# Splits moved on GpSimd and ScalarE, one load moved ahead, and the new part's weights in four groups of 32 columns from round 7 on

## The reference, cut to what matters

```
for t in range(768):                      # attention with a decaying state, B=2, H=8, D=48
    y[t]  = r[t] @ (state + (u*k[t]) v[t]^T)
    state = w[t][:,None]*state + k[t] v[t]^T
h = gelu(x @ w_in); u, v = halves of h    # stage 2, x is y as [2, 768, 384]
x1 = x + (u * (w_sg @ norm(v)*g_ln + b_sg)) @ w_out
x2 = x1 + (relu(x1^T @ tok1) @ tok2)^T    # stage 3
out = x2 + relu(x2 @ ch1) @ ch2
```

## Time and profile before

| what | us |
|---|---|
| time, median of 3 runs | 368.2 (368.17 to 368.8) |
| the profiled execution's own time | 369.53 |
| its span, first to last instruction | 368.0 |
| PE busy in the span | 359.9 |
| POOL busy | 188.6 |
| DVE busy | 163.0 |
| ACT busy | 106.6 |
| the six `xT` jobs that begin TAIL start at | 86.47 |

### The profile page before, as it was taken

One profiled execution on the slowest core, in us unless ns is written; L12 is line 12 of the kernel. 1 busy time (PEld: TensorE's weight loads), 2 busy tenths in 40 slices (PEclk: granted clock), 3 DMA queues, 4 the chain that ended last, 5 costly groups with the idle time before them and its releaser, 6 DMA issues.

```text
span 368.0 us, 6598 instructions
## 1 busy us (share of the span) xinstructions
PE 359.9 (98%) x2620; PEld 322.8 (88%) x2620; DVE 163.0 (44%) x272; ACT 106.6 (29%) x205; POOL 188.6 (51%) x191
## 2 busy tenths in 40 slices
PE   8999898999999999999999999999999999999996
PEld 8788787998999999999999998888888888888885
DVE  7989886656203323583469443340033300233100
ACT  3876267546450044310121312330022200132000
POOL 5997999999684465779999940037000000000000
PEclk9999999999999999999999999999999999999999
DMA  7985993311122000021223400000000000000011
GB/s 239 412 289 183 369 381 114 109 45 45 43 90 83 3 1 0 2 86 45 86 87 128 128 2 0 2 2 28 30 28 0 2 28 28 30 0 0 2 47 38
DMA packets 12463, 29.78 MB, mean 81 GB/s; under 512 B 1680, under 2 KB 5904, under 8 KB 12432
## 3 DMA queue, kind: packets, MB, share of 16 engines
q1 hardware_dynamic: 12432, 29.35, 22.8%
HBM read 26.99 MB, written 2.36 MB: 80 GB/s over the span
## 4 chain that ended last, share of the span: by engine, by line
PE 84%; POOL 8%; issue 3%; DVE 3%; ACT 1%; DVEq 0%; POOLq 0%
PE bank L1269 25%; PE bank L1268 25%; PE bank L1270 25%; PE bank L1291 2%; PE bank L1355 2%; PE bank L1454 2%; POOL sg_lo L621 1%; PE bank L1400 1%; POOL rp L677 1%; POOL rku L640 1%; POOL yt L693 1%; POOL rku L632 1%; POOL rstd L703 1%; PE bank L1301 1%; PE bank L1333 1%
## 5 line engine op out<-in xcount | busy, mean ns | idle before, releaser
L902 ACT ACTIVATE ha_hi<-bank 128x512 fp32r<-128x512 f32 x36 | 21.6, 601 | 106.6 <-PE bank L1270 106.6
L1176 DVE SCALAR_TENSOR_TENSOR ha_lo<-bank,ha_hi 128x512 fp32r<-128x512 f32 x36 | 24.9, 692 | 50.6 <-ACT ha_hi L902 50.6
L1268 PE MATMUL bank<-ha_hi,c_lo 128*128 128x512 f32 x108 | 42.1, 390 | 0.0
L1270 PE MATMUL bank<-u2T_hi,c_hi 128*128 128x512 f32 x108 | 42.0, 389 | 0.0
L1269 PE MATMUL bank<-u2T_lo,c_hi 128*128 128x512 f32 x108 | 42.0, 389 | 0.0
L1270 PE MATMUL bank<-ha_hi,c_hi 128*128 128x512 f32 x108 | 42.0, 389 | 0.0
L1269 PE MATMUL bank<-ha_lo,c_hi 128*128 128x512 f32 x108 | 42.0, 389 | 0.0
L1268 PE MATMUL bank<-u2T_hi,c_lo 128*128 128x512 f32 x108 | 42.0, 389 | 0.0
L1268 PE MATMUL bank<-sg_hi,z_lo 128*128 128x384 f32 x96 | 32.1, 334 | 0.0
L1269 PE MATMUL bank<-sg_lo,z_hi 128*128 128x384 f32 x96 | 32.1, 334 | 0.0
L1270 PE MATMUL bank<-sg_hi,z_hi 128*128 128x384 f32 x96 | 32.1, 334 | 0.0
(11 more groups left out here) (144 smaller groups left out, 833.6 us busy)
## 6 DMA issues: line engine op xcount, KB each, us to landing
turned<-in_turned_all SPq DMA_DIRECT2D x9, 772.0 KB, 7.7
raw<-in_moe_w_ch SPq DMA_DIRECT2D x12, 384.0 KB, 3.1
rows<-in_rows_all SPq DMA_DIRECT2D x6, 576.0 KB, 7.0
raw<-in_moe_w_sg SPq DMA_DIRECT2D x6, 384.0 KB, 3.0
out<-x2T SPq DMA_DIRECT2D x8, 256.0 KB, 2.0
raw<-in_moe_w_in SPq DMA_DIRECT2D x4, 384.0 KB, 5.0
raw<-in_moe_w_tok SPq DMA_DIRECT2D x4, 384.0 KB, 3.2
rows<-in_rows_all SPq DMA_DIRECT2D x6, 192.0 KB, 5.5
```

The source lines that it names most:

```text
L902: sc.activation(ha[0][:, i, :], bank[:, :], ACT.Relu).then_inc(act_out, 1)
L1176: ve.scalar_tensor_tensor(ha[1][:, i, :], bank[:, :], 0.0, ha[0][:, i, :].bitcast(F32), ALU.max, ALU.subtract).then_inc(dve_out, 1)
L1268: te.matmul(dst, left[1], right[0], start=first, stop=False)
L1270: return te.matmul(dst, left[0], right[0], start=False, stop=last)
```

## The change

Six edits:

- SP: the load `rows` of chunk 6 goes out ahead of the raw load of piece 2 (w_in 0), no longer behind it.
- The scaled r of round 0: POOL makes pair 0 only and DVE pairs 1 to 3 (before two and two). The scores of round 0 go through the pairs in the order 1, 2, 3, 0.
- POOL's low parts: w_in 1 moves from chunk 7 to 8, w_sg 0 from 8 to 9, w_sg 1 from 9 to 10, w_sg 2 from 10 to the work after the rounds.
- In chunk 11 POOL's `rstd_tile` comes behind `diagonal_v`, and ACT's `normal` for the same tile moves from round 11 to behind the last `xT` of TAIL.
- ACT's high part of w_in 0 moves from the end of round 5 into round 6, behind its `xT` job.
- PE: from round 7 on the new part takes the masked scores in four groups of 32 columns, so a round has 64 instructions at this line.

```diff
             load_raw(1)
+            load_rows(6)
             load_raw(2)
-            load_rows(6)
...
-            low = {6: [("w_in", 0)], 7: [("w_in", 1)], 8: [("w_sg", 0)], 9: [("w_sg", 1)], 10: [("w_sg", 2)]}
+            low = {6: [("w_in", 0)], 8: [("w_in", 1)], 9: [("w_sg", 0)], 10: [("w_sg", 1)]}
...
-                if len(last) == 1:
+                early = len(last) == 1 and n < NCH - 1
+                if early:
                     rstd_tile(*last[0])
...
                 diagonal_v(n)
-                if len(last) > 1:
+                if not early:
                     for b, i in last:
                         rstd_tile(b, i)
...
-                for i in range(3, NC):
+                for i in range(2, NC):
                     split_low("w_sg", i)
...
+                if n == YR + 1:
+                    split_high("w_in", 0)
                 if n % NC < NC - 1:
                     take_state(n)
...
-                if len(last) == 1:
+                if len(last) == 1 and n < NCH - 1:
                     normal(*last[0])
...
+                if (kind, b, i) == ("xT", 1, NC - 1):
+                    normal(*v_jobs(NCH - 2)[0])
...
-                ve.tensor_tensor(rp[0:QP, 0, 2:NP, :], kr_tile(0, 1)[:, 2:NP, :], pre_tile()[:, 2:NP, :], ALU.mult
+                ve.tensor_tensor(rp[0:QP, 0, 1:NP, :], kr_tile(0, 1)[:, 1:NP, :], pre_tile()[:, 1:NP, :], ALU.mult
...
+            quarters = [tile(i, HP // 2) for i in range(4)]
...
-                    for q in halves:
+                    for q in quarters if n > YR + 1 else halves:
                         ins = te.matmul(y_bank(n)[q, tile(h, D)], am[:, h, q], v_row(n)[:, tile(h, D)],
```

More of the change, by code:

```diff
@@ L667, in scale_first_r @@
                 pool.wait_ge(pre0_half, 1)
-                gp.tensor_tensor(rp[0:QP, 0, 0:2, :], kr_tile(0, 1)[:, 0:2, :], pre_tile()[:, 0:2, :], ALU.mult
+                gp.tensor_tensor(rp[0:QP, 0, 0:1, :], kr_tile(0, 1)[:, 0:1, :], pre_tile()[:, 0:1, :], ALU.mult
                                  ).then_inc(rp0_half, 1)
@@ L936, in split_high @@
                 sc.copy(hi, raw_view(piece, hi)).then_inc(w_hi_act, 1)
-            high = {5: [("w_in", 0)], 6: [("w_in", 1)], 7: [("w_sg", 0)], 8: [("w_sg", 1)],
+            high = {7: [("w_sg", 0)], 8: [("w_sg", 1)],
                     9: [("w_sg", 2)]}
@@ L986, in _ @@
                     take_job(*job)
-                for piece in high[n]:
-                    split_high(*piece)
+            split_high("w_in", 1)
             for n in range(YR + 2, NCH):
@@ L1077, in scale_first_r @@
                 wait_r(dve, 0)
+                dve.wait_ge(pre0_half, 1)
                 dve.wait_ge(pre_done, 1)
-                ve.tensor_tensor(rp[0:QP, 0, 2:NP, :], kr_tile(0, 1)[:, 2:NP, :], pre_tile()[:, 2:NP, :], ALU.mult
+                ve.tensor_tensor(rp[0:QP, 0, 1:NP, :], kr_tile(0, 1)[:, 1:NP, :], pre_tile()[:, 1:NP, :], ALU.mult
                                  ).then_inc(rp_done, 1)
@@ L1285, in scores @@
                     pe.wait_ge(masked, 2 * n)
-                for p in (range(NP) if n else (2, 3, 0, 1)):
+                for p in (range(NP) if n else (1, 2, 3, 0)):
                     if n == 0 and p == 0:
```

## The result

The changed kernel takes 366.79 us (median of 5 runs, 366.53 to 366.94), the kernel before 368.8 beside it (5 runs, 368.17 to 369.44). The ratio is 0.9948, 95% interval 0.9935 to 0.9961: 1.9 us faster by the ratio, 2.0 between the medians. Forecast was 365.8, with a range of 364.4 to 368.6. The profiled execution took 366.67 us, its span is 365.1.

A forecast was written before the change was run, and what follows sets the result against it. PE was taken as the bound, by how early it reaches TAIL. Terms -0.95, -1.15, -0.41, 0 and 0 made -2.5 us, the new part -1.0 + 1.1: -2.4, from 368.2 to 365.8 us; range 364.4 to 368.6.

The forecast's parts named there:

- the splits: POOL's low parts one chunk later: the stop ahead of round 9's scores goes, gain 1.15 us.
- the load of rows 6: Issued ahead of raw piece 2, it shortens PE's stop in round 6; gain 0.95 us, between 0.5 and 1.2.
- What bounds it: PE holds 84% of the chain of waits; the question is how early it reaches TAIL; three stops total 2.78 us.
- The lower bound of 1.3 us: Least gain in the landing of rows 6: one long raw-load issue of 1.70 us against 0.37, about 1.3 us.
- rival D: Stops come back elsewhere: rows 6 gains too little or rows 10 comes late; half of 2.5 left, 367.0 us; chance 0.13.
- rstd and normal: Moved out of round 11: PE's wait ahead of TAIL's first v job goes, gain 0.41 us.
- Round 0 and ACT's split: DVE's larger product in round 0 and ACT's later split of w_in 0: taken as 0, round 0 within -0.2 and +0.2.
- The new part: Four groups side by side in rounds 7 to 11: -1.0 us; nine changes of tile shape at 0.12: +1.1 us.
- A: New part's four groups run only two by two: +2.6 us, 368.3 us in all; chance 0.17.
- B: Each new-part instruction still costs 28.8 ns: +4.6 us, 370.3 us, up to 371.4; chance 0.13.
- C: New part's four groups run side by side, with no price for the change of shape: 364.7 us; chance 0.20.

The follow-up runs named there:

- the second look: The kernel before, run and profiled again with no edit: 368.45 us, span 366.9; the new part of round 6 starts at 38.56.

## Why the prediction was right, and where not

The measured time lies in the range. What was gained came by the splits and the lead that they give POOL; the second largest term, the load of rows 6, had next to nothing behind it.

- *What bounds it.* Right: the time went by how early PE reached TAIL, and from there on both kernels run alike.
- *The load of rows 6, -0.95.* Wrong. "The load `rows` of chunk 6" was late in the execution profiled, not in the kernel: the second look, the edit undone (367.02) and the changed kernel all start the new part of round 6 at 38.6. Its worth by the undone edit is 0 to 0.2 us. The lower bound of 1.3 us failed too: the long second issue went over to the load of rows, which ended 0.2 us sooner. One execution of 369.53 us, 1.3 above its median, was the sign, and I used it only to shift the sum. That is the first condition of rival D (the load gains too little), and by the absolute time D's 367.0 is nearer to 366.79 than the forecast's 365.8. By the gain it is not: 2.0 us measured, 2.4 forecast, 1.25 in D.
- *The splits, -1.15.* Right: 1.1 by undoing it, and 62.93 - 61.79 = 1.14 in the start of round 9's scores. POOL's `rp` ended at 61.08, 0.7 ahead of them, 1.0 said.
- *rstd and normal, -0.41.* Right that the edit removes the stop, since it does so with the splits back in their old chunks. But the splits alone remove it too, by POOL's lead of 2 to 3 us, which the same text had worked out; so the edit adds nothing to them (366.73 with it undone). The size was 0.66 by the distance of starts.
- *Round 0 and ACT's split, 0.* Right for round 0; DVE's product took 0.81 us, not 0.65. ACT's split was not tested by itself.
- *The new part, -1.0 + 1.1 = 0.* Right in both terms. Four side by side: a period of 42.5 ns (45 said), 0.68 us for the step alone. The change of shape: 0.10 and 0.17 for a pair, 0.12 each said. In all +0.03 a round, undone 366.95 against 366.79. The Trainium skill's rule ("TensorEngine Tiling (Array Packing)", Key Properties), that a change of mode drains TensorE, agrees in so far as going between 64 and 32 columns costs about 0.13 us a time; that it is a drain no run shows. Its floor of 25 ns between starts ("TensorE: Matmul & The Clock Gate", Wait — 56ns, not 53.3ns?) does not hold for tiles side by side: 64 starts in 0.68 us are 10.6 ns apart. Rivals A and B fall by that number, C by the price of the shape.
- *Sum.* Said -2.4, measured -2.0 (0.65% to 0.39%, 1.4 to 2.4 us). Between the two usual executions (spans 366.9 and 365.1) it is 1.8, round 9's 1.15 and TAIL's 0.66; the rest is scatter or what the load brings in other executions. Two of my terms are off in opposite ways: 0.95 that was not there, 0.25 too little at TAIL. That the time still fell into the range is owed to its width, and partly to luck: two errors of unlike sign. The rest of the 1.0 us by which 365.8 was too low is the kernel before itself, 368.2 in the three runs shown and 368.8 in the five beside the changed one. Of the chances, 0.70 for faster already holds all of D, so D has no part left in the 0.13 for no change.

## What to carry to other kernels

Before pricing a stop that ends with a DMA, ask whether the profiled execution is a usual one: if it lies above the median by the length of the stop, the stop may be that execution's alone. Where two edits free the same engine, work out each with the other in place, and undo them one at a time: an edit whose undoing changes nothing may still be enough by itself. Narrow groups on TensorE paid when neighbouring steps had the same shape (366.08 us here against 366.79 with one step alone). In the early rounds, where the loads are, the same groups cost 5.9 us (new part alone) and 16.4 us (all steps) against the changed kernel.

## What was not expected of the hardware

TensorE stood still, mostly in the middle of steps, in stops of 0.7 to 4.3 us at multiples of some 125 matmuls, when the rounds up to 6 had 32 or up to 80 more weight loads each. The places fit the borders of 16 KB instruction packets; the data transfers of these rounds are the suspected reason, but the DMA share in the stops ran from 0.01 to 1.00. The same groups of 32 columns from round 7 on cause none. Groups of 32 columns start some 10.6 ns apart: four side by side take 42.5 ns, where 48 moving columns in two passes at 2.4 GHz would be 40.
